# A fused attention and two feed-forward layers: feed-forward products begin one step earlier, in a reordered attention

## The reference

```python
def _attn_ref(q, k, v):                     # 4 x 8 heads x 576 x 64, factor = 4
    q_d, k_d, v_d = (x.reshape(B, H, S // 4, 4, D).mean(axis=3) for x in (q, k, v))
    out_up = np.repeat(sm_attn(q_d, k_d, v_d), 4, axis=2)
    mask = np.abs(pos[:, None] - pos[None, :]) < 4
    scores = np.where(mask, scale * q @ k.T, -1e9)
    return out_up + softmax(scores) @ v
def _moe_ref(x, w_in, w_out, alpha):        # 2304 tokens, 512 -> 2048 -> 512
    h = x @ w_in
    return (np.maximum(h, 0) + alpha * np.minimum(h, 0)) @ w_out
def _moe2_ref(x, w_in, w_out):              # with elu in place of prelu
    ...
```

## Time and profile before

| | us |
|---|---|
| three executions | 909.98, 911.39, 916.1 |
| median | 911.39 |
| the profiled execution | 912.4 |
| its span, first to last instruction | 910.6 |
| mean granted clock of PE in it | 0.996 of full speed |

### The profile page before, as it was taken

One profiled execution on the slowest core, in us unless ns is written; L12 is line 12 of the kernel. 1 busy time (PEld: TensorE's weight loads), 2 busy tenths in 40 slices (PEclk: granted clock), 3 DMA queues, 4 the chain that ended last, 5 costly groups with the idle time before them and its releaser, 6 DMA issues.

```text
span 910.6 us, 16928 instructions
## 1 busy us (share of the span) xinstructions
PE 897.1 (99%) x6508; PEld 832.1 (91%) x6508; DVE 538.1 (59%) x1049; ACT 299.1 (33%) x688; POOL 282.4 (31%) x406
## 2 busy tenths in 40 slices
PE   8889999999999999999999999999999999999998
PEld 5779999999999999999999998889888888888887
DVE  6675657555654454464465476566765657665563
ACT  5542324322422132242232233233432325423233
POOL 5689992111201235365376531100011100000000
PEclk9899999999999999999999999999999999999999
DMA  7775532222201125436262254434453444634411
GB/s 155 164 170 148 146 102 68 55 55 55 55 3 27 44 71 166 146 109 189 96 231 70 58 155 113 127 109 119 132 173 116 117 116 116 188 114 118 117 45 70
DMA packets 119840, 100.80 MB, mean 111 GB/s; under 512 B 66001, under 2 KB 82385, under 8 KB 119761
## 3 DMA queue, kind: packets, MB, share of 16 engines
q1 hardware_dynamic: 110512, 93.13, 37.2%
q10 hardware_dynamic: 9248, 6.59, 2.5%
HBM read 80.29 MB, written 19.40 MB: 109 GB/s over the span
## 4 chain that ended last, share of the span: by engine, by line
PE 94%; POOL 2%; issue 1%; DVE 1%; DMA 0%; SPq 0%; ACT 0%; DVEq 0%; POOLq 0%
PE ps L239 29%; PE ps L240 28%; PE ps L241 28%; PE ps L442 1%; PE ps L509 1%; PE ps L466 1%; PE ps L497 1%; PE ps L453 1%; PE ps L474 1%; PE ps L482 1%; POOL p_ls L695 1%; PE ps L1044 0%; DMA qk_nat<-in_k 0%; POOL p_cs L692 0%; PE ps L462 0%
## 5 line engine op out<-in xcount | busy, mean ns | idle before, releaser
L241 PE MATMUL ps<-common,w_hi 128*128 128x384 f32 x768 | 258.2, 336 | 0.0
L240 PE MATMUL ps<-common,w_hi 128*128 128x384 f32 x768 | 258.1, 336 | 0.0
L240 PEld LDWEIGHTS ps<-common,w_hi 128*128 128x128 f32 x768 | 144.6, 188 | 0.0
L241 PEld LDWEIGHTS ps<-common,w_hi 128*128 128x128 f32 x768 | 144.3, 188 | 0.0
L239 PE MATMUL ps<-common,w_out_lo 128*128 128x384 f32 x384 | 132.8, 346 | 0.2 <-DVE common L318 0.2
L239 PE MATMUL ps<-common,w_in_lo 128*128 128x384 f32 x384 | 132.5, 345 | 0.0
L314 ACT ACTIVATE common<-act_g 128x384 fp32r<-128x384 f32 x96 | 50.5, 526 | 242.3 <-PE ps L241 125.6
L872 ACT ACTIVATE act_g<-act_g 128x384 f32<-128x384 f32 x96 | 50.5, 526 | 195.1 <-DVE act_g L868 195.1
L239 PE MATMUL ps<-w_hi,common 128*128 128x512 f32 x288 | 113.6, 394 | 0.0
L241 PE MATMUL ps<-w_hi,common 128*128 128x512 f32 x288 | 113.5, 394 | 0.0
L240 PE MATMUL ps<-w_out_lo,common 128*128 128x512 f32 x288 | 113.5, 394 | 0.0
(11 more groups left out here) (100 smaller groups left out, 1418.7 us busy)
## 6 DMA issues: line engine op xcount, KB each, us to landing
ring<-w_in_parts SPq DMA_DIRECT2D x168, 256.0 KB, 2.7
w_in_parts<-parts SPq DMA_DIRECT2D x8, 1280.0 KB, 5.7
qk_nat<-in_q SPq DMA_DIRECT2D x32, 144.0 KB, 3.1
v_nat<-in_v SPq DMA_DIRECT2D x16, 288.0 KB
out<-xT SPq DMA_DIRECT2D x18, 256.0 KB, 2.2
qk_nat<-in_k SPq DMA_DIRECT2D x30, 144.0 KB, 3.3
v_win<-in_v SPq DMA_DIRECT2D x64, 67.5 KB
raw<-in_moe_w_in SPq DMA_DIRECT2D x16, 256.0 KB, 6.4
```

The costliest lines, as they stand in the source:

```text
L240: pe.matmul(psum, l_hi, r_lo, start=False, stop=False)
L241: return pe.matmul(psum, l_hi, r_hi, start=False, stop=stop)
```

## The change

Five things are changed together.

1. Rounds are two units in front in place of three, and a step is rounds, transposes, scores (local ones first), outputs.
2. The stretch in which attention runs alone ends behind the fourth unit's transposes, in the third step, in place of behind its outputs. The first lead now has the fourth unit's outputs, the fifth's transposes and the sixth's rounds; the second lead has the sixth's two local scores. Of the jobs that stood ahead of the first product, the sixth unit's rounds and scores, the seventh's rounds and the fourth's outputs stand behind it. Two of the eight filler matmuls go.
3. All eight banks are used in turn while attention is alone.
4. q and k have two places until the sixth unit; the second lies in xT, in the part of the second batch, so the loads of the first two units wait for nothing, and later ones for the unit two before.
5. w_in and w_out of a chunk are split by two functions with a semaphore each. POOL splits w_in of chunks 0 and 1 first, w_out of both behind the fifth unit's normalisation. The first product waits for w_in alone, the second for w_out.

The work of DVE and ACT moves with it: ACT takes the coarse exponentials a job later, DVE the reciprocals three jobs behind the coarse score.

```diff
-    SCORES = [("SC", 0), ("SL", 0), ("SL", 1)]
+    TRANSPOSES = [("TC", 0), ("TC", 1), ("TL", 0), ("TL", 1)]
+    SCORES = [("SL", 0), ("SL", 1), ("SC", 0)]
     OUTPUTS = [("O", 0), ("O", 1)]
-    STEP = [("TC", 0), ("TC", 1), ("TL", 0), ("TL", 1), *SCORES, *ROUNDS, *OUTPUTS]
-    AHEAD_OF = {"TC": 0, "TL": 0, "O": 0, "SC": 2, "SL": 2, "R": 3}
+    STEP = [*ROUNDS, *TRANSPOSES, *SCORES, *OUTPUTS]
+    AHEAD_OF = {"TC": 0, "TL": 0, "O": 0, "SC": 2, "SL": 2, "R": 2}
+    LAST_ALONE = BATCH_UNITS - 1
+    def jobs_of(jobs, u):
+        return [(*job, u) for job in jobs]
     def step_jobs(u):
         return [(kind, i, u + AHEAD_OF[kind]) for kind, i in STEP if u + AHEAD_OF[kind] < UNITS]
-    FIRST_SCORES = [("SL", 0), ("SL", 1), ("SC", 0)]
-    prologue = [(*job, u) for u in range(2) for job in ROUNDS + FIRST_SCORES] + [(*job, 2) for job in ROUNDS]
-    order = prologue + [job for u in range(UNITS) for job in step_jobs(u)]
-    ALONE = len(prologue) + BATCH_UNITS * len(STEP)
+    prologue = [job for u in range(2) for job in jobs_of(ROUNDS + SCORES, u)]
+    alone = prologue + [job for u in range(LAST_ALONE) for job in step_jobs(u)] + jobs_of(TRANSPOSES, LAST_ALONE)
+    leads = [jobs_of(OUTPUTS, LAST_ALONE) + jobs_of(TRANSPOSES, LAST_ALONE + 1) + jobs_of(ROUNDS, LAST_ALONE + 2),
+             jobs_of(SCORES[:2], LAST_ALONE + 2)]
+    behind_leads = jobs_of(SCORES[2:], LAST_ALONE + 2) + jobs_of(ROUNDS + SCORES, LAST_ALONE + 3) \
+        + jobs_of(OUTPUTS, LAST_ALONE + 1)
+    order = alone + sum(leads, []) + behind_leads + [job for u in range(LAST_ALONE + 2, UNITS) for job in step_jobs(u)]
+    ALONE = len(alone)
+    LEAD = [len(jobs) for jobs in leads]
     number = {job: n for n, job in enumerate(order)}
-    LEAD = [4, len(SCORES), 1]
+    assert len(number) == len(order) == UNITS * len(STEP)
+    FIRST_BANKS = [*range(4), 4, 5, 6, *range(4), 4, 5, 7, *range(4), 6, 4, 5, 0, 1, 2, 3, 7, 6]
+    RING_OF_BANKS = [4, 5, 0, 1, 2, 3, 7, 6]
+    LEAD_BANKS = [7, 6, *range(4), *range(4), 7, 6]
     def bank_of(kind, i, u):
         n = number[kind, i, u]
-        if ALONE <= n < ALONE + sum(LEAD):
-            return (3, 0, 1, 2, 3, 7, 6, 7)[n - ALONE]
-        if n >= ALONE:
-            return 6 + (n - ALONE - sum(LEAD)) % 2
-        if u == BATCH_UNITS - 1 and (kind, i) in OUTPUTS:
-            return (7, 6)[i]
-        if kind in ("TC", "TL", "R"):
-            return i + 2 * (kind == "TL")
-        if u < 2 and kind in ("SC", "SL"):
-            return 4 + {("SL", 0): 0, ("SL", 1): 1, ("SC", 0): 2}[kind, i]
-        step, place = (u - 2, SCORES.index((kind, i))) if kind in ("SC", "SL") else (u, OUTPUTS.index((kind, i)) + 1)
-        return 4 + (step + place) % 3
+        if n < len(FIRST_BANKS):
+            return FIRST_BANKS[n]
+        if n < ALONE:
+            return RING_OF_BANKS[(n - len(FIRST_BANKS)) % 8]
+        if n < ALONE + sum(LEAD):
+            return LEAD_BANKS[n - ALONE]
+        return 7 - (n - ALONE - sum(LEAD)) % 2
...
+        def behind_outputs_of(u):
+            return number["O", 1, u] + 1
+        first = behind_outputs_of(BATCH_UNITS * (t + 1) - 1) if t else ALONE
+        jobs = order[first:behind_outputs_of(BATCH_UNITS * (t + 2) - 1)]
+        sizes = [] if t else LEAD
         grouped = [jobs[sum(sizes[:n]):sum(sizes[:n + 1])] for n in range(len(sizes))]
         burst = []
         for job in jobs[sum(sizes):]:
-            if len(burst) == 2 or burst and job[1:3] == OUTPUTS[0]:
+            if len(burst) == 2 or burst and job[0:2] == OUTPUTS[0]:
...
-                    pe.wait_ge(w_split, c + 1)
+                    pe.wait_ge(w_in_split, c + 1)
...
+                if T == 0:
+                    pe.wait_ge(w_out_split, c + 1)
...
-            qk_nat = sb("qk_nat", [NP, 2, NT, HEADS, D])
+            qk_even = sb("qk_even", [NP, 2, NT, HEADS, D])
+            QK_SETS = LAST_ALONE + 3
+            QK_BLOCKS = 2 * NT * HEADS * D // (KC * XW)
+            qk_odd = xT[0:NP, 2 * NXB - QK_BLOCKS:2 * NXB, :, :].rearrange("p w k q -> p (w k q)")\
+                .rearrange("p (n t h d) -> p n t h d", n=2, t=NT, h=HEADS)
...
+            def qk_place(u):
+                return u % 2 if u < QK_SETS else 0
+            def qk_nat(u):
+                return qk_odd if qk_place(u) else qk_even
+            def loads_of(u):
+                return sum(qk_place(v) == qk_place(u) for v in range(u + 1))
...
+            def scored_at(n):
+                return order[n][2] if 0 <= n and order[n][0] == "SC" else None
             def act_job(act, kind, i, u):
                 if kind == "R":
                     copy_round(act, u, i)
-                    if i == 0:
-                        exp_local(act, u - 1, 1)
                 elif kind == "TC":
                     copy_pT_coarse(act, u, i)
                 elif kind == "TL":
                     copy_pT_local(act, u, i)
-                elif kind == "SL" and i == 0:
-                    exp_coarse(act, u)
-                elif kind == "SL":
+                elif kind == "SL" and i == 1:
                     exp_local(act, u, 0)
-                elif (kind, i) == OUTPUTS[0] and u + 2 == UNITS - 1:
-                    exp_local(act, u + 2, 1)
+                elif kind == "SC":
+                    exp_local(act, u, 1)
+                scored = scored_at(number[kind, i, u] - 1)
+                if scored is not None:
+                    exp_coarse(act, scored)
+                if (kind, i) == TRANSPOSES[-1] and 1 <= u <= BATCH_UNITS:
+                    act.wait_ge(x_done, 2 * u)
+                    split_x_hi(act, 0, u - 1)
...
             def dve_job(dve, kind, i, u):
+                n = number[kind, i, u]
+                if scored_at(n - 1) is not None:
+                    sum_local(dve, scored_at(n - 1), 1)
                 if kind == "SC":
                     max_coarse(dve, u)
+                    sum_local(dve, u, 0)
                 elif kind == "SL":
                     subtract_max(dve, u, i)
                 elif kind == "R":
                     pool_round(dve, u, i)
-                    if i == 1:
-                        sum_local(dve, u - 1, 0)
                 elif kind == "O":
                     if i == 0:
-                        if u + 2 < UNITS:
-                            if u + 3 == UNITS:
-                                sum_local(dve, u + 2, 0)
-                            sum_local(dve, u + 2, 1)
-                            reciprocals(dve, u + 2)
                         copy_coarse(dve, u)
                     write_x(dve, u, i)
+                if scored_at(n - 3) is not None:
+                    reciprocals(dve, scored_at(n - 3))
+                for v in range(BATCH_UNITS):
+                    scores = ("SL", 1, v + 3)
+                    if (kind, i, u) == (scores if number[scores] < ALONE else (*TRANSPOSES[-1], v + 1)):
+                        split_x_lo(dve, 0, v)
...
-            EARLY = BATCH_UNITS // 2
-            LATE = [range(n, min(n + 4, FC)) for n in range(EARLY, FC, 4)]
-            assert len(LATE) == BATCH_UNITS
+            WEIGHTS_BETWEEN = {BATCH_UNITS: (2, 1, 2), BATCH_UNITS + 1: (0, 0, 4), BATCH_UNITS + 2: (0, 0, 4),
+                               BATCH_UNITS + 3: (0, 0, 1)}
...
                     if u + 1 < UNITS:
                         sp.wait_ge(vd_done, u + 1)
                         load_v_nat(sp, u + 1)
-                    if u + 4 < UNITS:
-                        sp.wait_ge(r_done, 4 * (u + 3) + 2)
-                        load_q(sp, u + 4)
-                        sp.wait_ge(r_done, 4 * (u + 3) + 4)
-                        load_k(sp, u + 4)
-                    if u + 1 < WS:
-                        load_chunk(sp, u + 1)
+                    if u < 2:
+                        load_chunk(sp, u)
+                    elif u == LAST_ALONE:
+                        load_chunk(sp, 2)
+                    v = u + 4 if u < LAST_ALONE - 1 else u + 3
+                    had = v - 2 if v <= QK_SETS else v - 1
+                    if u != LAST_ALONE - 1 and v < UNITS:
+                        sp.wait_ge(r_done, 4 * had + 2)
+                        load_q(sp, v)
+                        sp.wait_ge(r_done, 4 * had + 4)
+                        load_k(sp, v)
...
+                sum_v(gp, 1)
+                normalise(gp, 2)
+                split_w_in(gp, 0)
+                sum_v(gp, 2)
+                normalise(gp, 3)
+                split_w_in(gp, 1)
+                sum_v(gp, 3)
+                normalise(gp, 4)
+                for c in range(2):
+                    split_w_out(gp, c)
```

More of the change, by code:

```diff
@@ L164, in bursts @@
     def bursts(t):
-        jobs = [(u, *job) for u in range(BATCH_UNITS * (t + 1), BATCH_UNITS * (t + 2)) for job in step_jobs(u)]
-        sizes = LEAD if t == 0 else []
+        def behind_outputs_of(u):
[3 more added lines that the diff above has]
+        sizes = [] if t else LEAD
```

(18 more changed lines are left out.)

153 lines of the change are left out of this document (71 added, 82 removed).

## The result

The changed kernel takes 929.29 us (median of four executions, 925.91 to 931.13). The kernel before took 911.93 beside it (909.98 to 916.1). The ratio is 1.018, with a 95% interval of 1.013 to 1.023. The forecast was 902.7 us, its range 899.1 to 906.5, and slower had a chance of 0.05.

What follows compares the result with a forecast made beforehand. PE, busy 897 of 910.6 us, bounds the kernel, with DVE holding the attention-alone stretch. M moves 10.4 us, less 1.9 deferred, plus 0.2: gain 8.7, so 903.7 profiled, 902.7 median; range 899.1 to 906.5.

Steps and rivals of the forecast that it cites:

- Behind M, PE is dense in both kernels: After the first second product: PE never idles, so the gain is M's shift, less deferred work, plus or minus stalls.
- M: Start of the first second product (c=0, m=0), the prediction's measuring point: 62.70 us in the kernel before.
- the 0.4 us for jobs: Behind M: 0.4 us counted for the coarse score and first round, which need the two local scores' banks.
- a slower kernel through a wait in the mix: Mixed stretch: second products wait 0.60 us at each of 16 chunks in two tiles, 19.2 us in, 921.9; chance 0.05.
- Deferred work: Moved behind M: the sixth unit's coarse score, 0.8 to 0.95 us, and the seventh unit's rounds, 1.1; together 1.9.
- M': Start of the first second product in the changed kernel: predicted 52.3, so it moves by 10.4 us.
- The start: Early attention-alone stretch: the third unit's local scores reach DVE at 20.6 us, bounds 20.0 and 21.6.
- The steps behind: Attention-alone stretch on DVE: fourth unit's scores 6.5 us after the third's, at 27.1; fifth's 7.2 later, at 34.3.
- a fall only after 47.5: Rival for 47.5 to 52.3, PE busy about 2.9 of 4.8 us: clock falls, 2.95 us lost, 905.7; chance 0.06.
- the windows of v, costed at nothing: Loads before a unit's outputs: ready 5.3 us after the previous outputs end, needed after 6 or more; 0.7 us spare.
- the three waits: PE waits of about 1, 1 and 1.8 us at the third product, the fourth unit's products and M'.
- The two subtractions of x: Low halves of the third and fourth units' x before the first products: 1.0 us each, beside POOL; without lock 0.55.

## Why the prediction was wrong

**The step that failed** is the sentence "Behind M, PE is dense in both kernels", and with it the 0.4 us for jobs "which need the banks of the two local scores". I looked for the new bank neighbours only at the first jobs behind M. The same two-bank alternation goes on for every later unit, and there the second output meets the coarse score. Measured: nine waits, 11.5 us, and 5.1 us of clock behind them. There was also a wait of 1.72 us for the copy kT at 64.51, which the prediction did not have either. One rival was a slower kernel through a wait in the mix, but I put it at DVE and the second products, and gave it 0.05 because DVE was only busy 39 of 64 us. Busy share was the wrong thing to look at: ACT is busy 32% of the span, and it idled 3.48 us in front of the late call. In an engine that works in order, what counts is what stands in front.

**Deferred work** was mis-sized: 1.9 us by the prediction, 4.45 by count. I had the coarse score of the sixth unit and the seventh unit's rounds, and missed the seventh unit's local and coarse scores, which the kernel before does ahead of M. With this alone the forecast gain of 8.7 would have been about 6.

**M'** was 55.17, predicted 52.3. The start was right: the third unit's local scores reach DVE at 20.67 (20.6). The steps behind were longer. DVE in the kernel after:

```profile
20.67 0.50 DVE L646 TENSOR_REDUCE stats<-ps 112x6 f32<-112x324 f32 x1
...
28.83 0.50 DVE L646 TENSOR_REDUCE stats<-ps 112x6 f32<-112x324 f32 x1 [0.28 <-PE ps L498]
...
36.50 0.49 DVE L646 TENSOR_REDUCE stats<-ps 112x6 f32<-112x324 f32 x1
```

8.2 and 7.7 us, where I had 6.5 and 7.2. PE's timeline from the second of these steps to M:

```profile
32.06 0.92 PE L541 MATMUL ps<-pT_l,v_win 54*64 54x48 f32 x48 [1.18 <-issue]
...
39.81 0.92 PE L541 MATMUL ps<-pT_l,v_win 54*64 54x48 f32 x48 [1.45 <-issue]
...
43.74 0.45 PE L254 MATMUL ps<-common,w_in_lo 128*128 128x384 f32 x1 [0.47 <-DVE common L313]
...
50.48 0.45 PE L254 MATMUL ps<-common,w_in_lo 128*128 128x384 f32 x1 [0.58 <-DVE common L313]
...
55.17 0.41 PE L254 MATMUL ps<-common,w_out_lo 128*128 128x384 f32 x1 [1.83 <-DVE common L335]
```

The first step is 1.7 us over. The clock was low from 20 to 25 us, 0.66 of full speed (1.7 us lost), behind two waits of PE of 0.88 and 0.92, and DVE waited for PE four times in this step, 1.7 us in all. I had looked for a fall only after 47.5, where there was none; and by my own ledger that stretch had 2.5 us of PE's work in it, not the 2.9 that I compared.

The second step is 0.5 over, and the stretch from the fifth unit's scores to the low half of x another 0.5. In each of them the windows of v, costed at nothing with 0.7 us to spare, came late: 1.18 and 1.45 us. I had 5.3 us from the end of the outputs before to the next ones and 6 or more between them. PE was ready 5.4 us behind that end both times, and the windows took 6.6 and 6.8. For the first, SP's queue began at once (25.55, outputs over at 25.49), and the last of the windows came 4.2 us behind its issue; why so late is not shown. For the second, the queue was still issuing k when the outputs were over (to 34.04, against 32.98), and the kernels with the third unit's windows in front of q and k show what that costs: 1.60 to 0.25.

**Right** were the three waits at the third product, the fourth unit's products and M' in place, and the last in size; the other two were about half of what I had (0.47, 0.58 and 1.83 us; predicted 1, 1 and 1.8). The two subtractions of x took 0.56 and 0.61 us, not the 1.0 that I took. They did not run alone: a sum on POOL beside the first took 0.93 us where its neighbours took 0.73, and a pair beside the second 1.74 where 1.42 is usual, so what I had charged to DVE may have fallen on POOL. No wait for q and none for weights was right too. (The range's upper bound, with its own terms, is 906.7 and not 906.5; that changes nothing.)

**What the change is worth without its slip**: nothing that can be measured (1.0012), until the issues are moved as well (0.9958). M is 4.2 to 7.5 us earlier (three executions of this alone stretch), 4.45 come back as deferred work, and the falls behind M and the wait for kT take the rest.

## What to carry to other kernels

When a change alters the order of jobs over a short cycle of banks, write down for *each* job of the steady step which job had its bank before and what stands in front of that job's reader in the reader's own queue; look at the steady part first, since what is lost there comes back every step. When work is started earlier, count instructions behind the measuring point in both kernels before calling the shift a gain. And ahead of rebuilding an order, look at what a queue issues in front of a late load: two places and two moved chunk loads in the kernel before gave more than the whole change.

## What the runs showed of the hardware

In the mix, the granted clock fell to its 1.2 GHz level soon behind single waits of 1.4 to 1.8 us in an otherwise dense stream, and each fall lost 1.5 to 1.7 us (in the changed kernel and in the one with the exponentials early). But it did not fall behind each of them: in the changed kernel it fell behind the waits that end at 74.33 (1.61 us), 101.00 (1.61) and 152.56 (1.39), and not behind those that end at 55.17 (1.83), 64.51 (1.72), 127.69 (1.61) and 252.57 (1.39). In the kernel with the exponentials early it did fall behind the waits at M and for kT (1.82 and 1.65 us), which are the places where it held in the changed kernel. I can't say from these runs what decides. The Trainium skill, "TensorE: Matmul & The Clock Gate", section "A second HAM failure mode: psum-queue depth-cycling", says that frequent short idle times of PE between groups of matmuls, as it goes round the banks, can send the clock down and up again. The trace agrees that short waits for a bank can do it (5.1 us lost in three falls), and differs from the page's case: here each fall stands behind one wait, and these waits are some 25 us apart.

In the changed kernel the nine waits were 11.5 us and the falls 5.1, so a wait for a bank in this mix cost about 1.4 times its length. And where the clock falls in the alone stretch, M shifts by a few microseconds between executions with the same alone stretch; a ledger that adds up single executions can be no finer than that.
